# Reordered steps ahead of two chunks, GpSimd subtractions in pieces of 256 columns, and identity turns on TensorE

## Chip, cores and metric

The kernel runs on one core of a Trainium2 chip. The metric is the device time of one execution in microseconds (us), here the median of three runs.

## What is computed

Batch 4, 8 heads, 576 tokens, head width 64, model width 512. Local attention, a gated channel mix, a token mix of rank 32 and a two-layer network follow one another. Cut to what matters:

```python
# attention: plain window of 32 keys for heads 0-3, every 4th of 128 keys for heads 4-7
scores = where(masks, q @ k.T / sqrt(64), -1e9)
attn   = exp(scores - max); attn = attn / (sum(attn) + 1e-9)
x      = attn @ v                                   # [4, 576, 512]
# channel mix, widths 512 -> 1024 -> 512
x_prev = x shifted by one token (0 first)
xk = mu_k * x + (1 - mu_k) * x_prev
xr = mu_r * x + (1 - mu_r) * x_prev
x  = sigmoid(xr @ w_r) * (relu(xk @ w_k) ** 2 @ w_v)
# token mix of rank 32, then a network 512 -> 2048 -> 512
u   = x + (x.T @ U @ V).T
out = u + relu(u @ w_ch1) @ w_ch2
```

## The kernel before

Every matrix product of the two networks is made of three products of rounded parts: high by high, low by high, high by low (`three`, L1172 to L1174). So each operand has a high half (a rounded copy, made by ScalarE or GpSimd) and a low half (operand minus high half, made by VectorE or GpSimd).

**Attention** goes by parts and pairs. A part k is half a batch (256 or 320 tokens), a pair p two heads; "(1, 2)" is part 1, pair 2. Each has four steps:
- A: VectorE turns q and k in blocks of 32 (L951, L959).
- B: TensorE makes the scores (L1193, L1206); VectorE masks them and takes the maximum (L973, L979, L983); ScalarE takes the exponentials (`exps`, L720); VectorE normalises (`normalise`, L1006 to L1011).
- C: TensorE turns the probabilities against an identity matrix (L1213); ScalarE copies them out (L710).
- D: TensorE multiplies by v (L1224); VectorE copies the result into `x` (L993 to L997).

Part 0 and the scores of (1, 0) run ahead of everything, in the order of the list `BEFORE`; the others are dealt to slots by the tables `FIRST_ONE`, `SECOND_ONE` and `LATER`. Each engine's program writes its order out by hand.

**Channel mix** goes by nine chunks of 256 tokens. A chunk has ten units on TensorE, one slot of attention behind each: k units (128 columns of `xk @ w_k`) and two r units (128 tokens of `xr @ w_r`), in the order k0, k1, k2, r0, r1, k3 to k7. Behind some units stand the products with `w_v` (`V_AFTER`), which need the square of a k unit: ScalarE makes relu and the rounded square, VectorE the square (`sq`, L1030) and its low half (`sq_l`, L1034).

For the first chunk the k mix is made pair by pair: ScalarE shifts (`first_shift`), VectorE mixes (`mix`, L1020), ScalarE rounds (`high_first`), VectorE makes the low half (`low_first`, L1103). The r mix is made by GpSimd (`mix_r`, L633), rounded by ScalarE (`high_first_r`, L784), and its low half made by GpSimd (`low_first`, L644). In later chunks GpSimd makes the low half of the r mix in one instruction (`low_xr`, L628).

**Weights** come in pieces of 512 KB (`load_piece`); the first ten are split into halves by GpSimd (`split_both`, L621 and L622). Piece 0 serves k0 and k1, piece 1 k2 and k3, pieces 2 and 3 the r units, piece 4 the first products with `w_v`. The pieces of the last network are rounded by ScalarE and subtracted by GpSimd (`split_low`, L613).

**Queues.** SyncE issues q, v, most weights and a part of k, in program order, each load waiting for its buffer. ScalarE issues seven loads of k (`load_keys`). GpSimd goes through its splits, mixes and low halves in program order.

Of the kernel before, what the change touches and what calls it, by code (L numbers as in the profile page):

```python
# [30 lines left out]
D = H * DH  # L31
# [51 lines left out]
def blocks(k, p):  # L83
# [8 lines left out]
          ("D", 0, 2), ("C", 0, 3), ("D", 0, 3), ("B", 1, 0)]  # L92
NUNIT = 10

LATER = {"A": [-7, -5, -2, 0], "B": [-6, -4, -1, 1], "C": [-2, 0, 3, 5], "D": [-1, 1, 4, 6]}
FIRST_ONE = {"A": [None, None, 1, 2], "B": [None, 0, 1, 3], "C": [1, 3, 4, 5], "D": [2, 4, 5, 6]}
# [108 lines left out]
def build(nc, q, k_in, v, mu_k, mu_r, w_k, w_v, w_r, u_in, v_in, w_ch1, w_ch2, out):  # L205
    ctx = ExitStack()
    with ctx:
# [160 lines left out]
        def wait(eng, s, value):  # L368

            value = value + CREDIT.get(id(s), 0)  # L370
            if isinstance(value, int) and value <= 0:
                return
            eng.wait_ge(s, value)
# [13 lines left out]
        def two_of(step):  # L387
            return two_banks[TWO[GROUP[step]]]
# [67 lines left out]
        def _(sp):  # L456
# [71 lines left out]
            load_qk(0, 0)  # L528
            load_qk(0, 1)
            load_v(0, 0)  # L530
            load_qk(0, 2)
            load_piece(0)
            load_v(0, 1)
            load_qk(0, 3)
            load_piece(1)
# [3 lines left out]
            load_piece(2)  # L539
# [35 lines left out]
        def _(pool):  # L575
# [33 lines left out]
            def split_low(n):  # L609

                raw, hi, lo = piece(n)
                pool.wait_ge(w_hi, n - FIRST2 + 1)
                pool.tensor_tensor(lo, raw, hi.bitcast(F32), ALU.subtract).then_inc(w_split, 1)  # L613

            def split_both(n):

                raw, hi, lo = piece(n)
                pool.wait_ge(stage_in[slot_of(n)], STAGE_COUNT[n])
                half = raw.shape[1] // 2
                for a in (slice(0, half), slice(half, 2 * half)):  # L620
                    step(pool.tensor_copy(hi[:, a], raw[:, a]))  # L621
                    ins = pool.tensor_tensor(lo[:, a], raw[:, a], hi[:, a].bitcast(F32), ALU.subtract)  # L622
                ins.then_inc(w_split, 1)

            def low_xr(c):

                wait(pool, xrh_done, c + 2)
                pool.tensor_tensor(xs_l[:, 1], xf[:, 1], xs_h[:, 1].bitcast(F32), ALU.subtract).then_inc(xrl_done, 1)  # L628
# [12 lines left out]
            def low_first(half):  # L641
                wait(pool, xrh_done, half + 1)
                f = HEAD_PAIR[2 * half]
                return pool.tensor_tensor(xs_l[:, 1, f:f + 2], xf[:, 1, f:f + 2], xs_h[:, 1, f:f + 2].bitcast(F32), ALU.subtract)  # L644
# [18 lines left out]
            low_first(0)  # L663
            low_first(1).then_inc(xrl_done, 1)
            for n in range(4, NB_PIECES):
                split_both(n)
# [35 lines left out]
        def _(act):  # L702
# [110 lines left out]
            def chunk(c):  # L813
                last = c == NC1 - 1
                for n, (kind, m) in enumerate(UNITS):
# [12 lines left out]
                    if c == 0 and n == 2:  # L828
                        high_first_r(0)
                        high_first_r(1)  # L830
                    if n == NUNIT - 2 and c > 0 and not last:
                        high_x(1, c + 1)
                    if c < MIX_CHUNK:
                        attention_slot(c * NUNIT + n)
                    else:
                        for step in mix_steps("scalar", (c - MIX_CHUNK) * NUNIT + n):
                            mix_step(*step)
# [16 lines left out]
            def first_exps(k, p):  # L854
                exps(k, p, 0)
                exps(k, p, 1)
# [22 lines left out]
            load_keys(1, 0, range(2, 4))  # L879
            first_exps(0, 3)  # L880
            first_shift(1)
            attention("C", 0, 2)
            high_first(1)
            load_keys(1, 1)
            first_shift(2)
            attention("C", 0, 3)
# [4 lines left out]
            shift_for_r(0, 1)  # L891
            load_keys(1, 2)
            shift_for_r(0, 2)
# [34 lines left out]
        def _(dve):  # L928
# [140 lines left out]
            def chunk(c):  # L1069
                last = c == NC1 - 1  # L1070
                slot = c * NUNIT
                for n, (kind, m) in enumerate(UNITS):
                    if n >= 1 and UNITS[n - 1][0] == "k":
                        square(c, UNITS[n - 1][1])
                    for t in range(KT):
                        if not last and n == MIX_SLOT[c][t]:
                            mix(c + 1, t)
                    if c < MIX_CHUNK:
                        for step in steps_in(slot + n):
                            attention(*step)  # L1080
                        for k, p in normalised_in(slot + n):
                            normalise(k, p)
                    else:
                        for step in mix_steps("vector", (c - MIX_CHUNK) * NUNIT + n):
                            mix_step(*step)
# [37 lines left out]
            low_first(0)  # L1123
            mix(0, 1)
            normalise(0, 3)
            attention("D", 0, 2)
            low_first(1)
            mix(0, 2)
            attention("A", 1, 0)
# [5 lines left out]
            attention("A", 1, 1)  # L1135
            for c in range(NC1):
                chunk(c)
# [29 lines left out]
        def _(pe):  # L1167
# [7 lines left out]

            def attention(stage_, k, p):
# [5 lines left out]
                dst, run = two_of((stage_, k, p)), run_of((stage_, k, p))  # L1182
                every = units(k, p)
# [23 lines left out]
                elif stage_ == "C":  # L1207
                    if n == 0:
                        pe.wait_ge(consts, 1)
# [121 lines left out]

            pe.wait_ge(cleared, 2)
            for step in BEFORE:
                attention(*step)
            for n in range(len(BEFORE)):
                if TWO[n] < 2 and TWO[n] not in TWO[n + 1:]:
                    wait_drained(pe, GROUPS[n])
            for c in range(NC1):
                chunk(c)
# [65 lines left out]
```

## Time and profile before

| | |
|---|---|
| runs | 789.57, 789.8, 791.19 us; median 789.8 us |
| profiled execution | 787.75 us, of which the span from the first to the last instruction is 785.7 us |
| mean granted TensorE clock | 0.996 of full speed |
| busy | TensorE 95%, its weight loads 83%, VectorE 43%, ScalarE 38%, GpSimd 19% |
| DMA | 35.75 MB in 121746 packets |

Busy shares are means over stages with different limits: the first 50 us, with attention of part 0 and the first chunk, look different from the rest. In rows of the trace a time is counted from the start of the span. PE is TensorE, DVE VectorE, ACT ScalarE, POOL GpSimd, SP SyncE; SPq is SyncE's queue of DMA issues. In rows in order of time a bracket gives the idle time of the engine just ahead of the instruction, and what ended it.

### The profile page before, as it was taken

The page shows a single profiled execution, that of the slowest core. Times are in us where ns is not written, and L with a number is a line of the kernel's source. Part 1 is how long each engine was busy: PE and PEld are TensorE (multiplying, and loading weights), DVE is VectorE, ACT ScalarE, POOL GpSimd, SP SyncE. Part 2 cuts the span into 40 slices and gives each one's busy share as a digit, 9 for nine tenths or more (in the row PEclk, how much of TensorE's full clock was granted, in tenths as well). Part 3 has the DMA queues.
Part 4 walks back from the last instruction along what each step waited for, and adds up shares of the span by engine and source line. Part 5 has one row for each costly group of instructions (what it writes and reads, how often), then busy time and mean ns, then how long its engine had stood idle before and what let it go on. Part 6 is the DMA issues. An engine that isn't in the chain of part 4 may idle for free.

```text
span 785.7 us, 13228 instructions
## 1 busy us (share of the span) xinstructions
PE 749.7 (95%) x5020; PEld 655.0 (83%) x5020; DVE 334.5 (43%) x704; ACT 295.6 (38%) x777; POOL 149.9 (19%) x163
## 2 busy tenths in 40 slices
PE   4589899999999999989999999999999999999998
PEld 3467788888888887779889999899998989989997
DVE  6768776767676846755411311221131122113111
ACT  4657676666777665612532211111111111112110
POOL 5777220102011215200665000000000000000000
PEclk9989999999999999999999999999999999999999
DMA  7963342333233201000342100010010001001001
GB/s 143 208 155 61 65 82 48 60 57 70 42 59 62 56 1 54 1 27 1 113 143 67 41 0 1 1 40 0 0 40 0 0 0 40 0 0 41 0 1 41
DMA packets 121746, 35.75 MB, mean 46 GB/s; under 512 B 109536, under 2 KB 115680, under 8 KB 121696
## 3 DMA queue, kind: packets, MB, share of 16 engines
q1 hardware_dynamic: 112000, 34.02, 17.9%
q10 hardware_dynamic: 9696, 1.05, 0.9%
q8 instruction: 32, 0.52, 0.3%
q14 instruction: 18, 0.15, 0.1%
HBM read 30.33 MB, written 4.72 MB: 45 GB/s over the span
## 4 chain that ended last, share of the span: by engine, by line
PE 88%; DVE 7%; issue 2%; ACT 2%; ACTq 0%; POOL 0%; DMA 0%; DVEq 0%
PE bank L1172 27%; PE bank L1174 26%; PE bank L1173 26%; PE bank L1224 2%; PE bank L1193 2%; PE bank L1213 2%; DVE sq L1030 1%; PE bank L1253 1%; DVE xf L1020 1%; DVE probs L973 1%; PE bank L1314 1%; DVE sq_l L1034 1%; ACT probs L720 1%; DVE neg_max L983 1%; PE bank L1326 0%
## 5 line engine op out<-in xcount | busy, mean ns | idle before, releaser
L1142 DVE SCALAR_TENSOR_TENSOR h_l<-bank,h_h 128x384 fp32r<-128x384 f32 x96 | 53.5, 558 | 305.6 <-ACT h_h L912 305.5
L912 ACT ACTIVATE h_h<-bank 128x384 fp32r<-128x384 f32 x96 | 47.2, 492 | 330.7 <-PE bank L1174 330.7
L1172 PE MATMUL bank<-ut_h,w_h 128*128 128x384 f32 x384 | 130.6, 340 | 0.7 <-POOL w_l L613 0.7
L1174 PE MATMUL bank<-ut_h,w_l 128*128 128x384 f32 x384 | 129.3, 337 | 0.0
L1173 PE MATMUL bank<-ut_l,w_h 128*128 128x384 f32 x384 | 128.8, 336 | 0.0
L1174 PE MATMUL bank<-w_h,h_l 128*128 128x512 f32 x288 | 113.7, 395 | 0.0
L1173 PE MATMUL bank<-w_l,h_h 128*128 128x512 f32 x288 | 113.5, 394 | 0.0
L1172 PE MATMUL bank<-w_h,h_h 128*128 128x512 f32 x288 | 112.0, 389 | 0.0
L1172 PE MATMUL bank<-xs_h,wk_h 128*128 128x256 f32 x288 | 85.6, 297 | 1.9 <-DVE xs_l L1103 1.9
L1173 PE MATMUL bank<-xs_l,wk_h 128*128 128x256 f32 x288 | 81.1, 282 | 0.0
L1174 PE MATMUL bank<-xs_h,wk_l 128*128 128x256 f32 x288 | 80.9, 281 | 0.0
L1172 PEld LDWEIGHTS bank<-ut_h,w_h 128*128 128x128 f32 x384 | 72.2, 188 | 4.9 <-POOL w_l L613 1.0
L1173 PEld LDWEIGHTS bank<-ut_l,w_h 128*128 128x128 f32 x384 | 72.2, 188 | 3.0
L1174 PEld LDWEIGHTS bank<-ut_h,w_l 128*128 128x128 f32 x384 | 72.0, 188 | 0.0
L1172 PE MATMUL bank<-wv_h,sq_h 128*128 128x512 f32 x144 | 58.8, 408 | 5.1 <-DVE sq_l L1034 5.0
L1174 PEld LDWEIGHTS bank<-w_h,h_l 128*128 128x128 f32 x288 | 54.0, 188 | 11.5
L1173 PEld LDWEIGHTS bank<-w_l,h_h 128*128 128x128 f32 x288 | 54.0, 188 | 9.5
L1172 PEld LDWEIGHTS bank<-w_h,h_h 128*128 128x128 f32 x288 | 54.1, 188 | 9.0
L819 ACT ACTIVATE relu_k<-bank 128x256 f32<-128x256 f32 x72 | 27.0, 375 | 90.7 <-PE bank L1174 90.6
L1172 PEld LDWEIGHTS bank<-xs_h,wk_h 128*128 128x128 f32 x288 | 54.8, 190 | 5.8 <-issue 3.3
L1173 PE MATMUL bank<-wv_l,sq_h 128*128 128x512 f32 x144 | 57.0, 396 | 0.0
L1174 PE MATMUL bank<-wv_h,sq_l 128*128 128x512 f32 x144 | 56.9, 395 | 0.0
(118 smaller groups left out, 1211.9 us busy)
## 6 DMA issues: line engine op xcount, KB each, us to landing
stage<-in_moe_w_ch_dram SPq DMA_DIRECT2D x16, 512.0 KB, 3.4
out_dram<-result SPq DMA_DIRECT2D x18, 256.0 KB, 2.0
q_raw<-in_q_dram SPq DMA_DIRECT2D x64, 40.0 KB, 2.1
q_raw<-in_q_dram SPq DMA_DIRECT2D x64, 32.0 KB, 2.1
v_raw<-in_v_dram SPq DMA_DIRECT2D x32, 64.0 KB, 2.4
k_raw<-in_k_dram SPq DMA_DIRECT2D x48, 40.0 KB, 2.1
k_raw<-in_k_dram SPq DMA_DIRECT2D x52, 32.0 KB, 2.1
stage<-in_moe_w_k_dram SPq DMA_DIRECT2D x3, 512.0 KB, 4.1
```

Of the source, the lines that this page charges most:

```text
L720: ins = act.activation(probs[b][:, keys * i:keys * i + keys], probs[b][:, keys * i:keys * i + keys], ACT.Exp, bias=neg_max[:, b, i:i + 1], ...
L819: act.activation(relu_k[:, m % 2, :], unit_bank[n % 2][:, 0:C1], ACT.Relu).then_inc(unit_out, 1)
L912: act.activation(h_h[:, m % KRING, :], h_bank[m % 2][:, 0:C2], ACT.Relu).then_inc(hh_done, 1)
L973: ins = dve.scalar_tensor_tensor(probs[b][:, 0:4 * keys].rearrange("p (h c) -> p h c", h=2), banks[:, :, 0:2 * keys], DH ** -0.5, m[:, :, ...
L983: dve.tensor_reduce(neg_max[:, b, 0:nu], probs[b][:, 0:nu * keys].rearrange("p (a b) -> p a b", b=keys), op=ALU.max, axis=AX_X, negate=Tru ...
L1142: dve.scalar_tensor_tensor(h_l[:, m % KRING, :], h_bank[m % 2][:, 0:C2], 0.0, h_h[:, m % KRING, :].bitcast(F32), op0=ALU.max, op1=ALU.subt ...
L1172: pe.matmul(dst, lhs[0], rhs[0], start=start, stop=False)
L1173: pe.matmul(dst, lhs[0], rhs[1], start=False, stop=False)
L1174: return pe.matmul(dst, lhs[1], rhs[0], start=False, stop=stop)
L1193: ins = pe.matmul(dst[UQ * a:UQ * a + UQ, h, col:col + keys], q_t[n % 2][rows, query:query + UQ], k_t[p][rows, first_key:first_key + keys] ...
L1213: ins = pe.transpose(run[0:keys, i * P:i * P + P], probs[n % 2][:, keys * i:keys * i + keys], ident[:, :])
L1224: ins = pe.matmul(run[rows, to:to + wide], v_raw[n % VALUES][0:keys, i + a, rows], probs_t[n % 2][0:keys, block_, first:first + wide], sta ...
```

## The change

- `FIRST_ONE`: step A of (1, 2) goes ahead of chunk 0, and that of (1, 3) from slot 2 to slot 1.
- SyncE: pieces 0, 1 and 2 are loaded earlier than some loads of q and v.
- GpSimd: subtractions go in pieces of 256 columns (`split_low`, `split_both`, `low_xr`, `low_first`), and piece 4 is split ahead of the low half of the first r mix.
- ScalarE: other order of the steps ahead of chunk 0; in chunk 0 `high_first_r` goes from behind the relu of unit 2 to behind the attention slot of unit 1.
- VectorE: other order ahead of chunk 0; in chunk 0 (1, 0) is normalised ahead of the scores of (1, 1).
- TensorE: `keep_clock` turns the identity matrix into a bank that is free, 18, 12, 10, 6, 8, 3, 5 and 6 times ahead of seven attention steps and of chunk 0. It waits for the identity at the start.

```diff
+IDLE_TURNS = {("B", 0, 0): 18, ("B", 0, 1): 12, ("C", 0, 0): 10, ("B", 0, 3): 6, ("D", 0, 2): 8, ("C", 0, 3): 3, ("D", 0, 3): 5, "chunk": 6}
...
-FIRST_ONE = {"A": [None, None, 1, 2], "B": [None, 0, 1, 3], "C": [1, 3, 4, 5], "D": [2, 4, 5, 6]}
+FIRST_ONE = {"A": [None, None, None, 1], "B": [None, 0, 1, 3], "C": [1, 3, 4, 5], "D": [2, 4, 5, 6]}
...
             load_qk(0, 0)
+            load_piece(0)
             load_qk(0, 1)
             load_v(0, 0)
             load_qk(0, 2)
-            load_piece(0)
+            load_piece(1)
+            load_qk(0, 3)
             load_v(0, 1)
-            load_qk(0, 3)
-            load_piece(1)
+            load_piece(2)
             load_v(0, 2)
             load_v(0, 3)
             load_qk(1, 0)
-            load_piece(2)
             load_qk(1, 1)
             load_piece(3)
...
             def split_both(n):
...
-                half = raw.shape[1] // 2
-                for a in (slice(0, half), slice(half, 2 * half)):
+                raw, hi, lo = (a.rearrange("p t (z n) -> p (t z) n", n=256) for a in (raw, hi, lo))
+                for a in (slice(0, 2), slice(2, 4)):
                     step(pool.tensor_copy(hi[:, a], raw[:, a]))
-                    ins = pool.tensor_tensor(lo[:, a], raw[:, a], hi[:, a].bitcast(F32), ALU.subtract)
+                    for i in range(a.start, a.stop):
+                        ins = pool.tensor_tensor(lo[:, i], raw[:, i], hi[:, i].bitcast(F32), ALU.subtract)
...
             def low_xr(c):
 
                 wait(pool, xrh_done, c + 2)
-                pool.tensor_tensor(xs_l[:, 1], xf[:, 1], xs_h[:, 1].bitcast(F32), ALU.subtract).then_inc(xrl_done, 1)
+                for f in range(KT):
+                    ins = pool.tensor_tensor(xs_l[:, 1, f], xf[:, 1, f], xs_h[:, 1, f].bitcast(F32), ALU.subtract)
+                ins.then_inc(xrl_done, 1)
...
                 mix_r(0, t)
-            low_first(0)
-            low_first(1).then_inc(xrl_done, 1)
-            for n in range(4, NB_PIECES):
+            split_both(4)
+            for t in range(KT):
+                ins = low_first(t)
+            ins.then_inc(xrl_done, 1)
+            for n in range(5, NB_PIECES):
...
-                    if c == 0 and n == 2:
-                        high_first_r(0)
-                        high_first_r(1)
...
                         attention_slot(c * NUNIT + n)
+                        if c == 0 and n == 1:
+                            high_first_r(0)
+                            high_first_r(1)
...
             load_keys(1, 0, range(2, 4))
+            attention("C", 0, 2)
             first_exps(0, 3)
             first_shift(1)
-            attention("C", 0, 2)
+            load_keys(1, 1)
             high_first(1)
-            load_keys(1, 1)
+            attention("C", 0, 3)
             first_shift(2)
-            attention("C", 0, 3)
             high_first(2)
             shift_for_r(0, 0)
             first_shift(3)
             high_first(3)
             shift_for_r(0, 1)
+            shift_for_r(0, 2)
             load_keys(1, 2)
-            shift_for_r(0, 2)
...
                     if c < MIX_CHUNK:
+                        if slot + n == 0:
+                            normalise(1, 0)
                         for step in steps_in(slot + n):
                             attention(*step)
...
             low_first(0)
+            normalise(0, 3)
             mix(0, 1)
-            normalise(0, 3)
             attention("D", 0, 2)
             low_first(1)
+            attention("A", 1, 0)
             mix(0, 2)
-            attention("A", 1, 0)
...
             attention("A", 1, 1)
+            attention("A", 1, 2)
...
+            def keep_clock(ahead_of, scratch):
+                for _ in range(IDLE_TURNS.get(ahead_of, 0)):
+                    pe.transpose(scratch[:, 0:P], ident[:, :], ident[:, :])
...
                 dst, run = two_of((stage_, k, p)), run_of((stage_, k, p))
+                keep_clock((stage_, k, p), run)
...
+            pe.wait_ge(consts, 1)
             pe.wait_ge(cleared, 2)
...
+            keep_clock("chunk", unit_bank[0])
             for c in range(NC1):
                 chunk(c)
```

## Rows read from the trace of the kernel before

**Rows 1.** The page's busy times: us (share of the span) and instructions.

```profile
PE 749.7 (95%) x5020; PEld 655.0 (83%) x5020; DVE 334.5 (43%) x704; ACT 295.6 (38%) x777; POOL 149.9 (19%) x163
```

**Rows 2.** TensorE in order of time, 30 to 76 us: start, duration, instruction.

```profile
30.05 0.55 PE L1172 MATMUL bank<-xs_h,wk_h 128*128 128x256 f32 x1 [1.89 <-DVE xs_l L1103]
...
37.98 0.72 PE L1213 MATMUL bank<-ident,probs 128*96 128x128 f32 x5 [1.83 <-DVE probs L1011]
39.59 0.56 PE L1193 MATMUL bank<-k_t,q_t 64*64 64x96 f32 x16 [0.89 <-DVE k_t L951]
...
45.98 0.77 PE L1172 MATMUL bank<-wr_h,xs_h 128*128 128x512 f32 x1 [3.24 <-issue]
...
63.63 0.72 PE L1213 MATMUL bank<-ident,probs 128*96 128x128 f32 x5 [0.56 <-DVE probs L1011]
...
75.17 0.60 PE L1213 MATMUL bank<-ident,probs 128*64 128x128 f32 x4 [0.77 <-DVE probs L1011]
```

**Rows 3.** Windows: PE, PEld, DVE, ACT, POOL busy, then granted clock, DMA share, GB/s.

```profile
34.84:45.08 10.24, 5.18 (x72) 4.42 (x71) 8.91 (x24) 6.59 (x26) 4.18 (x6) 1.00 0.83 196
45.08:51.91 6.83, 5.93 (x14) 4.70 (x15) 3.45 (x3) 2.25 (x6) 6.59 (x7) 0.50 0.80 202
51.91:58.00 6.09, 6.09 (x46) 4.83 (x46) 3.44 (x8) 2.93 (x8) 5.85 (x7) 1.00 0.47 126
```

**Rows 4.** ScalarE in order of time: last exponential of (1, 1); the two roundings.

```profile
40.38 0.19 ACT L720 ACTIVATION_READ_ACCUMULATOR probs<-probs,neg_max 128x1 f32 x1
...
42.69 1.13 ACT L784 ACTIVATE xs_h<-xf 128x512 fp32r<-128x512 f32 x2
```

**Rows 5.** GpSimd in order of time: piece 3, r mix, its low half, piece 4.

```profile
30.88 0.61 POOL L621 CAST wr_h<-x 128x512 fp32r<-128x512 f32 x1
...
34.71 2.61 POOL L633 TENSOR_TENSOR xf<-xf,shifted 128x256 f32<-128x256 f32 x4
43.38 2.50 POOL L644 TENSOR_TENSOR xs_l<-xf,xs_h 128x512 fp32r<-128x512 f32 x2 [6.06 <-ACT xs_h L784]
45.82 1.04 POOL L621 CAST wv_h<-x 128x512 fp32r<-128x512 f32 x1
```

**Rows 6.** SyncE's queue in order of time: the issue of piece 3.

```profile
24.70 0.46 SPq L514 DMA_DIRECT2D x<-in_moe_w_r_dram  x1
```

**Rows 7.** DMA issues at 22 to 23 and 24.5 to 25 us: size, us to landing.

```profile
x<-in_moe_w_r_dram SPq DMA_DIRECT2D x1, 512.0 KB, 4.4
...
x<-in_moe_w_r_dram SPq DMA_DIRECT2D x1, 512.0 KB, 5.8
```

**Rows 8.** VectorE in order of time: q of (1, 0), q of (1, 2).

```profile
25.35 0.73 DVE L951 STREAM_TRANSPOSE q_t<-q_raw 128x256 f32<-128x256 f32 x2
...
38.55 0.50 DVE L951 STREAM_TRANSPOSE q_t<-q_raw 128x320 f32<-128x320 f32 x1
```

**Rows 9.** VectorE in order of time: squares and a low half.

```profile
80.12 2.59 DVE L1030 TENSOR_TENSOR sq<-relu_k 128x256 f32<-128x256 f32 x1
...
331.11 2.20 DVE L1030 TENSOR_TENSOR sq<-relu_k 128x256 f32<-128x256 f32 x1
333.35 2.52 DVE L1034 TENSOR_TENSOR sq_l<-sq,sq_h 128x256 fp32r<-128x256 f32 x1
...
336.38 0.41 DVE L1030 TENSOR_TENSOR sq<-relu_k 128x256 f32<-128x256 f32 x1
```

**Rows 10.** GpSimd in order of time, beside the rows before.

```profile
80.01 2.42 POOL L628 TENSOR_TENSOR xs_l<-xf,xs_h 128x1024 fp32r<-128x1024 f32 x1 [5.89 <-ACT xs_h L771]
...
330.63 2.41 POOL L628 TENSOR_TENSOR xs_l<-xf,xs_h 128x1024 fp32r<-128x1024 f32 x1 [1.17 <-ACT xs_h L771]
333.24 2.34 POOL L613 TENSOR_TENSOR w_l<-stage,w_h 128x1024 fp32r<-128x1024 f32 x1 [0.21 <-ACT w_h L738]
```

**Rows 11.** TensorE in order of time, at the same two places.

```profile
83.23 0.50 PE L1172 MATMUL bank<-wv_h,sq_h 128*128 128x512 f32 x1 [2.11 <-DVE sq_l L1034]
...
335.91 0.50 PE L1172 MATMUL bank<-wv_h,sq_h 128*128 128x512 f32 x1 [2.54 <-DVE sq_l L1034]
```

More of the change, by code:

```diff
@@ L612, in split_low @@
                 pool.wait_ge(w_hi, n - FIRST2 + 1)
-                pool.tensor_tensor(lo, raw, hi.bitcast(F32), ALU.subtract).then_inc(w_split, 1)
+                raw, hi, lo = (a.rearrange("p t (z n) -> p (t z) n", n=256) for a in (raw, hi, lo))
+                for i in range(4):
+                    ins = pool.tensor_tensor(lo[:, i], raw[:, i], hi[:, i].bitcast(F32), ALU.subtract)
+                ins.then_inc(w_split, 1)
             def split_both(n):
@@ L618, in split_both @@
                 pool.wait_ge(stage_in[slot_of(n)], STAGE_COUNT[n])
-                half = raw.shape[1] // 2
-                for a in (slice(0, half), slice(half, 2 * half)):
+                raw, hi, lo = (a.rearrange("p t (z n) -> p (t z) n", n=256) for a in (raw, hi, lo))
+                for a in (slice(0, 2), slice(2, 4)):
                     step(pool.tensor_copy(hi[:, a], raw[:, a]))
-                    ins = pool.tensor_tensor(lo[:, a], raw[:, a], hi[:, a].bitcast(F32), ALU.subtract)
+                    for i in range(a.start, a.stop):
+                        ins = pool.tensor_tensor(lo[:, i], raw[:, i], hi[:, i].bitcast(F32), ALU.subtract)
                 ins.then_inc(w_split, 1)
@@ L639, in make_xr, with low_first @@
                 low_xr(c)
[L641 to L644, printed above, removed]
+            def low_first(t):
+                wait(pool, xrh_done, t // 2 + 1)
+                f = HEAD_PAIR[t]
+                return pool.tensor_tensor(xs_l[:, 1, f], xf[:, 1, f], xs_h[:, 1, f].bitcast(F32), ALU.subtract)
             pool.memset(u_pad[:, :, :, :].rearrange("p a t r -> p (a t r)"), 0.0).then_inc(u_zero, 1)
@@ L1081, in chunk @@
                         for k, p in normalised_in(slot + n):
-                            normalise(k, p)
+                            if (k, p) != (1, 0):
+                                normalise(k, p)
                     else:
@@ L1207, in attention @@
                 elif stage_ == "C":
-                    if n == 0:
-                        pe.wait_ge(consts, 1)
                     wait(pe, normed, n + 1)
```

## The prediction

> **What bounds the kernel now.** I read the page's busy times first, then TensorE in order of time, then GpSimd, SyncE and ScalarE over the first 50 us, and at the end VectorE against GpSimd. TensorE is busy for 749.7 us of a 785.7 us span [rows 1]: 36.0 us are all that can be gained by removing its waits, and what a faster clock gives comes on top. The profiled execution took 787.75 us, 2.05 us less than the median of the three runs (789.8 us) and below the lowest of them. I work out differences on the profiled execution and take them off the median.
>
> The reader should look at TensorE's order of time [rows 2]. Chunk 0 begins at 30.05 us. Inside it TensorE waits 1.83 us for the normalised probabilities of part 1, pair 0, then 0.89 us for the turned q and k of pair 2, then 3.24 us ahead of the first r unit at 45.98 us. Behind that it waits 0.56 and 0.77 us at two turns of probabilities, and later twice for the low part of a square [rows 11]. The granted clock belongs to the same stretch [rows 3]: it is at 2.4 GHz (1.00) from 34.84 us, falls to 1.2 GHz (0.50) at 45.08 us, which is inside the gap of 3.24 us, and comes back at 51.91 us, after 5.93 us of work at half speed. That work lost 5.93 / 2 = 2.96 us.
>
> So the start of the first r unit is the place to price. What sets it? It needs the low half of the r mix. GpSimd made that at 43.38 us, after 6.06 us of waiting for ScalarE's rounding (high_first_r), which ran at 42.69 us because it stood behind the relu of unit 2 [rows 4, 5].
>
> **The first r unit after the change: 3.4 us earlier.** Two chains must both end.
>
> GpSimd's chain: its piece 3 is issued by SyncE at 24.70 us [rows 6]. Before piece 3 the queue holds the same loads in both kernels, piece 2 included, only in another order, so I leave the issue at 24.7. It landed 5.8 us after the issue; piece 2 landed 4.4 us after its own [rows 7]. With piece 2's 512 KB out of the way earlier, I take 4.8 us, landing at 29.5 us (bounds 29.1 and 30.5). Piece 3's split lasts from 30.88 to 34.71 us, 3.83 us [rows 5]; GpSimd waits for the data now, since the earlier pieces come early, so it ends at 33.4. Four mixing sums take 2.6 us [rows 5]: 36.0. The new order puts the split of piece 4 here, another 3.9 us with two more instructions: 39.9. Four low parts of 256 columns cost what four mixing sums of that size cost, 2.6 us: 42.5. The unit starts 0.1 us later, at 42.6.
>
> ScalarE's chain: the two roundings come behind the exponentials of pair 1, which end at 40.57 us in the trace of before [rows 4]. Chunk 0 starts about a microsecond earlier (below), so I expect them at about 39.5 to 40.6; at the old time they would end at 40.57 + 1.13 = 41.7 us [rows 4] and the unit would start at about 43.1. GpSimd's chain therefore decides, with 42.2 to 43.6 as bounds from the landing, and 44.0 if a rounding is late as well. The gain is 45.98 - 42.6 = 3.4 us, bounds 2.0 and 3.8.
>
> **Edits that I cost at nothing, and their cover.** Normalising pair 0 of part 1 ahead of pair 1's scores, and turning pair 2 ahead of the chunk, take away the 1.83 and 0.89 us waits. Even without them and with the old start TensorE would only reach the first r unit at (45.98 - 3.24) - 2.72 = 40.0 us, where it waits until 42.6: they are covered by GpSimd's chain, and would be worth 2.7 us if that chain ended first. The moved turn is one more thing that VectorE waits for: pair 2's k is loaded by ScalarE's queue after one more shift. The normalising, the scores and the squares of the chunk stand behind it. It was done at 38.55 us [rows 8], so a late landing has cover only while these stay ahead of ScalarE's roundings.
>
> In the preamble, piece 0 now goes ahead of q of pair 1, piece 1 ahead of q of pair 3 and piece 2 ahead of two loads of v. Each may hold the small loads for one transfer. The turn of part 1's first q and k goes ahead of mix 2 on VectorE; in the kernel before it ran at 25.35 us right behind that mix [rows 8], so its data had landed by then, and at worst VectorE waits for it until about 25.35. The mix, the turn and the low parts after it then end 0 to 1 us before the old time. So chunk 0 starts between 29.0 and 30.05 us. TensorE's slack of 2.6 us at the r unit covers all of this.
>
> The 68 identity turns: one turn costs 0.72 - 0.60 = 0.12 us at full clock (five turns against four [rows 2]) and twice that at half, together 8.2 to 16.3 us. They stand where TensorE waits, ahead of steps whose operands are late. Where a turn outlasts its wait (12 turns at half clock are 2.9 us) the preamble moves by some tenths, which VectorE's wait for q and k covers. The Trainium skill (TensorE: Matmul & The Clock Gate, Part 4: PE-mode transpose) says that transpose mode does not engage the full clock as other matmuls do. No row of the kernel before has turns alone ahead of a rise, so the trace shows neither. By that rule the sum is unchanged, since no term rests on the turns; without it the second case below would be likelier by about a tenth.
>
> **The clock at the r unit: nothing gained.** If TensorE reaches the r unit at 39 to 40 and starts at 42.6, it stands still for 2.6 to 3.6 us. The nearest row is the 3.24 us gap, in which the clock fell. I take the same half-speed stretch again: 0, with 2.96 us as the upper bound and a loss of 0.5 as the lower (a stretch that begins a little later relative to the unit).
>
> **GpSimd's subtractions in pieces of 256 columns: 4.1 us.** Beside GpSimd's 1024-column subtraction at 80.01 us (2.42 us), VectorE's square took 2.59 us [rows 9, 10], where the same shape takes 0.41 [rows 9]: 2.2 us of it were GpSimd's. TensorE then waited 2.11 us for the low part of that square [rows 11]. In four pieces a VectorE instruction is held for one piece, 2.42 / 4 = 0.6 us. Held on the square and again on its low part, VectorE still gains 2.2 - 1.2 = 1.0 us; held on neither, all 2.11. I take 1.3.
> At 331 us it happens twice in a row: the square takes 2.20 us beside one subtraction, its low part 2.52 beside the next [rows 9, 10], 3.9 us in excess. With at most 0.6 for each, 2.7 us go, more than TensorE's wait of 2.54 [rows 11]. I take 2.4 (1.5 to 2.54).
> The waits of 0.56 and 0.77 us [rows 2] end chains on VectorE in the stretch where GpSimd splits weights without a pause; with halved holds I take 0.4 of them (0 to 1.3). The added instructions cost GpSimd a few hundredths each, and it idles from there on.
>
> **Sum.** 3.4 + 0 + 1.3 + 2.4 + 0.4 = 7.5 us: 789.8 - 7.5 = 782.3 us. TensorE is busy almost throughout after the first r unit, so a shift there should survive to the end.
>
> **The rivals.** About 0.2% (1.6 us) is what a measurement of this kernel can tell from no change.
> - Half speed again at the r unit, as forecast: 782.3 us, its own range 780 to 785, chance 0.52.
> - The clock stays at 2.4 GHz through the gap, since the units before it are packed more closely: 2.96 us more, 779.3 us. For it: an idle stretch of 1.83 us in the kernel before did not lower the clock [rows 2, 3]. Against it: 3.24 did. Chance 0.26.
> - A new wait takes the place of the old one: pair 2's turn stands ahead of the chunk and its k lands late, VectorE's queue stands still, ScalarE's roundings slip to the old time, and the r unit starts near 45.5 us. Only the finer pieces remain: 789.8 - 4.1 - 0.5 = about 785.2 us. Chance 0.11.
> - No measurable change: VectorE is held by every piece in turn and nothing is gained at the squares, and what the r unit gains is given back to VectorE later in chunk 0. About 789 us, chance 0.06.
> - Slower: with the r unit earlier, waits between the next units keep the clock at 1.2 GHz through chunk 0. Each microsecond at half speed loses half a microsecond, so this eats the 7.5 us when the low stretch reaches 6.83 + 15 = 21.8 us, and is slower by 0.2% from 25 us on. A stretch of 31 us gives 789.8 - 7.5 + 12.1 = 794.4 us. Against it: in the kernel before the clock came back 5.93 us into the r unit although the stretch began idle [rows 3]. Chance 0.05.
>
> **How the numbers follow.** Faster by over 0.2%: 0.52 + 0.26 + 0.11 = 0.89; within 0.2%: 0.06; slower: 0.05. The range reaches down to the second case with larger gains at the squares (777.5 us) and up past the third (786 us); the last two cases, and the extreme ends of the others, are left out.
>
> **What would show it.** TensorE's first r unit should start at 42 to 44 us, released by GpSimd's low part; the piece ahead of it should be the split of piece 4. The waits of 1.83 and 0.89 us should be gone. The granted clock shows 0.50 somewhere between 42 and 52 us in the first case and not in the second. Squares near 77 and 326 us should take under 1.1 us. The prediction is wrong if the r unit starts after 45 us, if the waits for the low part of a square stay above 1.5 us, or if TensorE shows new waits of more than 2 us in chunk 0 or 1.

## The result and the profile after

The kernel after the change takes 783.78 us (median of five runs, 782.64 to 784.97), the kernel before beside it 790.93 us (789.57 to 792.81). The ratio is 0.991 [0.9889, 0.993], that is 7.1 us less. The profiled execution of after took 783.19 us, its span 781.4 us.

Busy times of after, to be read against [rows 1]:

```profile
PE 756.1 (97%) x5088; PEld 661.5 (85%) x5088; DVE 328.6 (42%) x704; ACT 295.2 (38%) x777; POOL 168.4 (22%) x257
```

TensorE has 68 instructions more, the turns. GpSimd has 94 more and is busy for 18.5 us longer. TensorE of after in order of time, against [rows 2, 11]:

```profile
31.04 0.39 PE L1187 MATMUL bank<-xs_h,wk_h 128*128 128x256 f32 x1 [1.59 <-DVE xs_l L1117]
...
38.90 0.72 PE L1231 MATMUL bank<-ident,probs 128*96 128x128 f32 x5 [2.54 <-DVE probs L1022]
...
46.94 0.77 PE L1187 MATMUL bank<-wr_h,xs_h 128*128 128x512 f32 x1 [2.49 <-issue]
...
63.10 0.72 PE L1231 MATMUL bank<-ident,probs 128*96 128x128 f32 x5 [0.39 <-DVE probs L1022]
...
73.84 0.60 PE L1231 MATMUL bank<-ident,probs 128*64 128x128 f32 x4 [0.17 <-DVE probs L1022]
...
80.69 0.50 PE L1187 MATMUL bank<-wv_h,sq_h 128*128 128x512 f32 x1 [0.89 <-DVE sq_l L1045]
```

The first r unit, which the forecast put at 42.6 us, starts at 46.94 us, a microsecond later than in the profile of before. The wait of 1.83 us for the probabilities of (1, 0) has not gone; it is now 2.54 us. Behind the r unit the waits shrink about as forecast: 0.56, 0.77 and 2.11 us have become 0.39, 0.17 and 0.89, and the 2.54 us near 335 us have no successor.

VectorE of after, in order of time, shows why the probabilities are late, and what the squares take, against [rows 8, 9]:

```profile
36.57 0.51 DVE L962 STREAM_TRANSPOSE q_t<-q_raw 128x320 f32<-128x320 f32 x1 [2.82 <-DMA k_raw<-in_k_dram]
37.01 0.47 DVE L962 STREAM_TRANSPOSE k_t<-k_raw 128x320 f32<-128x320 f32 x1
37.40 0.13 DVE L1017 TENSOR_SCALAR sums<-sums 128x5 f32<-128x5 f32 x1
...
78.80 0.97 DVE L1041 TENSOR_TENSOR sq<-relu_k 128x256 f32<-128x256 f32 x1
...
330.97 0.41 DVE L1041 TENSOR_TENSOR sq<-relu_k 128x256 f32<-128x256 f32 x1
331.42 0.85 DVE L1045 TENSOR_TENSOR sq_l<-sq,sq_h 128x256 fp32r<-128x256 f32 x1
```

The turn of (1, 2), which now stands ahead of the chunk, waits 2.82 us for k. The normalising of (1, 0) stands behind it and begins at 37.40 us. The three lower rows answer to squares of 2.59 and 2.20 us and a low half of 2.52 us before.

From there the delay goes through ScalarE to GpSimd. ScalarE's two roundings in after, then GpSimd, against [rows 4, 5]:

```profile
42.89 1.14 ACT L795 ACTIVATE xs_h<-xf 128x512 fp32r<-128x512 f32 x2
```

```profile
29.78 0.76 POOL L627 CAST wr_h<-x 128x512 fp32r<-128x512 f32 x1 [4.54 <-DMA x<-in_moe_w_r_dram]
...
34.28 2.61 POOL L642 TENSOR_TENSOR xf<-xf,shifted 128x256 f32<-128x256 f32 x4
...
39.97 1.59 POOL L629 TENSOR_TENSOR wv_l<-x,wv_h 128x256 fp32r<-128x256 f32 x2
43.58 3.26 POOL L653 TENSOR_TENSOR xs_l<-xf,xs_h 128x256 fp32r<-128x256 f32 x4 [2.02 <-ACT xs_h L795]
...
78.69 4.20 POOL L636 TENSOR_TENSOR xs_l<-xf,xs_h 128x256 fp32r<-128x256 f32 x4 [5.69 <-ACT xs_h L782]
```

GpSimd has done the split of piece 4 at 41.56 us and waits 2.02 us for the roundings. The last row is the subtraction that took 2.42 us in one instruction [rows 10]: in four pieces it takes 4.20 us. The shortest of the 32 pieces of this kind in after takes 0.72 us, so four of them would be 2.9 us; the other 1.3 us fall where VectorE works beside them, whose square and low half take 0.97 and 0.83 us there instead of 0.41 and 0.42.

How can the time fall by 7 us when the r unit starts later than in the profile of before? That profile isn't the typical execution. A second one has its first r unit at 48.31 us (below). Over the 59 executions of before that ran beside the experiments time goes roughly with the mean granted clock: 0.996 in seven of them, 788.3 us on average; 0.993 in 19, 789.9 us; 0.989 in seven, 791.8 us. The profile of before, with 0.996, is one of the short ones.

The table gives, for one profiled execution of each kernel, the start of the first and the second r unit of chunk 0, of the first r unit of chunk 1, and the rest of the span from there. Kernels are compared below by their ratios to runs of before on the same chip, with the 95% interval in brackets.

| kernel | r0 | r1 | r0 of chunk 1 | rest | span |
|---|---|---|---|---|---|
| before | 45.98 | 54.23 | 90.61 | 695.1 | 785.7 |
| before, again | 48.31 | 56.30 | 92.49 | 695.0 | 787.5 |
| after | 46.94 | 53.87 | 88.43 | 693.0 | 781.4 |
| e1 pieces only | 48.91 | 55.95 | 92.34 | 693.0 | 785.3 |
| e2 whole subtractions | 44.30 | 52.09 | 87.88 | 695.1 | 783.0 |
| e3 no turns | 46.20 | 54.22 | 88.74 | 692.9 | 781.6 |
| e7 turns only | 47.11 | 55.16 | 91.72 | 695.1 | 786.8 |
| e4 turn in slot 1 | 44.92 | 52.34 | 86.69 | 692.9 | 779.6 |
| e5 old loads | 47.34 | 55.47 | 90.09 | 692.9 | 783.0 |
| e6 both | 46.64 | 53.65 | 88.27 | 692.9 | 781.2 |
| e8 slot 1, more turns | 44.75 | 51.85 | 86.39 | 692.9 | 779.3 |
| e9 early keys | 44.82 | 52.53 | 86.52 | 693.0 | 779.5 |
| e10 keys and turns | 44.56 | 50.15 | 85.35 | 693.1 | 778.4 |
| e11 three edits | 43.17 | 50.68 | 86.78 | 693.0 | 779.8 |

Two things can be read off. The rest takes one of two values: 695.0 to 695.1 with whole subtractions (four profiles), 692.9 to 693.1 with pieces (ten), whatever else is changed. And against the second profile of before the 6.1 us of span are 1.4 up to the first r unit, 1.1 more up to the second, 1.6 up to chunk 1's, and 2.0 behind it.

### The profile page after: what moved, and what is told of

Same layout as the page of the kernel before. It is cut to its first block, busy times and chain, and to the rows that moved or that the text cites. A ratio compares the mean times of both kernels' runs of the same rounds, so it can differ in the third digit from the quotient of the medians.

```text
span 781.4 us, 13455 instructions
## 1 busy us (share of the span) xinstructions
PE 756.1 (97%) x5088; PEld 661.5 (85%) x5088; DVE 328.6 (42%) x704; ACT 295.2 (38%) x777; POOL 168.4 (22%) x257
## 4 chain that ended last, share of the span: by engine, by line
PE 88%; DVE 5%; issue 2%; ACT 2%; DMA 1%; SPq 0%; POOL 0%; ACTq 0%; DVEq 0%
PE bank L1187 27%; PE bank L1189 26%; PE bank L1188 26%; PE bank L1242 2%; PE bank L1231 2%; PE bank L1213 2%; PE bank L1271 1%; PE bank L1332 1%; DVE sq L1041 1%; DVE probs L984 1%; PE bank L1344 1%; DMA q_raw<-in_q_dram 1%; DMA k_raw<-in_k_dram 1%; ACT probs L731 1%; DVE sq_l L1045 0%
## 5 line engine op out<-in xcount | busy, mean ns | idle before, releaser
L618 POOL TENSOR_TENSOR w_l<-stage,w_h 128x256 fp32r<-128x256 f32 x64 | 47.7, 777 | 46.2 <-ACT w_h L749 46.1
```

The costliest lines, as they stand in the source:

```text
L618: ins = pool.tensor_tensor(lo[:, i], raw[:, i], hi[:, i].bitcast(F32), ALU.subtract)
```

## The experiments

The letters in the expectations stand for what is said to carry the gain or the wait: P the pieces, O the orders, T the turns on TensorE, C the clock at the r unit, W VectorE's wait for k of (1, 2), L the moved loads as the cause of a late start, G GpSimd's chain, S the three edits of e11 alone.

**Pieces alone (e1) and all but the pieces (e2).** e1 is the kernel before with the finer subtractions in `split_low`, `split_both`, `low_xr` and `low_first`; e2 is the kernel after with these four as before. The edit of e1, at one of the four places:

```diff
-                pool.tensor_tensor(lo, raw, hi.bitcast(F32), ALU.subtract).then_inc(w_split, 1)
+                raw, hi, lo = (a.rearrange("p t (z n) -> p (t z) n", n=256) for a in (raw, hi, lo))
+                for i in range(4):
+                    ins = pool.tensor_tensor(lo[:, i], raw[:, i], hi[:, i].bitcast(F32), ALU.subtract)
+                ins.then_inc(w_split, 1)
```

> The kernel before with one part of the change alone: GpSimd's subtractions in pieces of 256 columns. Theory P (the pieces carry the gain): TensorE's waits of 2.11 and 2.54 us at the squares shrink to under 1 us and 0, those of 0.56 and 0.77 us by about half, and the time falls by 4 to 5 us; the first r unit stays at about 46 us. Rival O (orders and turns carry it): less than 1.5 us faster, since VectorE is only held by the next piece instead.

> The changed kernel with GpSimd's subtractions whole again, all orders and turns as changed. Theory P: only 2 to 3 us faster than the kernel before, with both waits at the squares back at over 2 us. Rival O: 6 to 7 us faster, as the whole change.

Measured: e1 0.9961 [0.9945, 0.9977], 3.1 us faster; e2 0.9965 [0.9951, 0.9979], 2.8 us faster. So both halves of the change are real and of about one size. TensorE of e1, at new and old waits:

```profile
79.79 0.56 PE L1200 MATMUL bank<-k_t,q_t 64*64 64x96 f32 x16 [1.21 <-DVE k_t L958]
...
84.93 0.50 PE L1179 MATMUL bank<-wv_h,sq_h 128*128 128x512 f32 x1 [1.12 <-DVE sq_l L1041]
```

and of e2:

```profile
80.48 0.50 PE L1180 MATMUL bank<-wv_h,sq_h 128*128 128x512 f32 x1 [2.12 <-DVE sq_l L1038]
...
333.32 0.50 PE L1180 MATMUL bank<-wv_h,sq_h 128*128 128x512 f32 x1 [2.53 <-DVE sq_l L1038]
```

With whole subtractions both old waits are back to within a hundredth of a microsecond. With pieces the second has gone and the first is halved, but in e1 a wait of 1.21 us for a turn on VectorE takes the place of what the first gave: from the second r unit to chunk 1's, e1 takes 36.4 us and before 36.2 to 36.4.

**No turns (e3), and the turns alone in the kernel before (e7).**

```diff
-IDLE_TURNS = {("B", 0, 0): 18, ("B", 0, 1): 12, ("C", 0, 0): 10, ("B", 0, 3): 6, ("D", 0, 2): 8, ("C", 0, 3): 3, ("D", 0, 3): 5, "chunk": 6}
+IDLE_TURNS = {}
```

> The changed kernel without the 68 identity turns. Theory T (the turns raise the clock, which fell again twice near the first r unit): TensorE's steps before 30 us run at half speed, chunk 0 starts about 1 us later than with turns, and the kernel is 0.5 to 2 us slower than the changed one. Rival (the start of chunk 0 hangs on loads and VectorE alone, so the turns are worth nothing): within 0.5 us of the changed kernel.

> The kernel before with the 68 identity turns alone. Theory T: the granted clock is 1.00 from about 6 us on, chunk 0 starts 1 to 2 us earlier, the units k0 and k1 take 1.4 us each instead of 2.6 and 1.8, but the first r unit still waits for its low half, and the time falls by 1 to 2.5 us. Rival (worth nothing): within 0.8 us of the kernel before.

Measured: e3 783.2 us, 0.992 [0.9902, 0.9938], no different from after; e7 1.0005 [0.999, 1.002]. The turns are worth nothing that these runs can tell. They do act on TensorE, though. After, then e3, at the first steps:

```profile
1.54 4.10 PE L1193 MATMUL bank<-ident 128*128 128x128 f32 x18 [1.54 <-POOL ident L589]
6.73 0.46 PE L1213 MATMUL bank<-k_t,q_t 64*64 64x64 f32 x16 [1.09 <-DVE k_t L970]
7.12 1.53 PE L1193 MATMUL bank<-ident 128*128 128x128 f32 x12
```

```profile
5.76 0.71 PE L1213 MATMUL bank<-k_t,q_t 64*64 64x64 f32 x16 [5.76 <-DVE k_t L970]
```

18 turns with nothing beside them take 4.10 / 18 = 0.23 us each. The 16 scores behind them take 0.46 us, against 0.71 without turns, and the next twelve turns 0.13 us each. (That these scores start a microsecond later in after than in e3 is not the turns' doing: VectorE waits 4.26 us for the first k in after and 3.20 in e3, with the same loads.) But the scores begin when VectorE has turned k, and so does all that follows: a quarter of a microsecond gained in a chain that hangs on loads goes into the next wait. Chunk 0 starts at 29.97 us in e7, and at 30.05 and 30.16 in the two profiles of before.

**The wait for k (e4) and the moved loads (e5, e6), beside another profile of before.** e4 leaves the turn of (1, 2) in slot 1, as in the kernel before; e5 gives SyncE's loads their old order; e6 does both.

```diff
-FIRST_ONE = {"A": [None, None, None, 1], "B": [None, 0, 1, 3], "C": [1, 3, 4, 5], "D": [2, 4, 5, 6]}
+FIRST_ONE = {"A": [None, None, 1, 1], "B": [None, 0, 1, 3], "C": [1, 3, 4, 5], "D": [2, 4, 5, 6]}
...
             attention("A", 1, 1)
-            attention("A", 1, 2)
```

> The changed kernel with one edit taken back: q and k of part 1, pair 2 are turned in slot 1 of chunk 0 again and not ahead of the chunk (those of pair 3 stay in slot 1). Theory W (the new wait of VectorE for k of pair 2, 2.8 us in the trace of the changed kernel, is what ate the earlier start of the first r unit): the normalising of pair 0 starts about 2 us earlier, ScalarE's roundings end near 41 instead of 44 us, the first r unit starts at 44 to 45 us instead of 46.9, and the kernel is 1.5 to 2.5 us faster than the changed one. Rival G (GpSimd's own queue holds the r unit anyway): within 0.5 us of the changed kernel.

> The changed kernel with SyncE's loads in the order of before. Theory L (piece 0 ahead of the small loads made the first q and k land 1.1 to 2 us later): the first turn starts at 4.5 us instead of 5.6, the second at 7.4 instead of 9.3, chunk 0 starts near 29 us instead of 31.0, the first r unit at 44 to 45 us, and the kernel is 1.5 to 3 us faster than the changed one. Rival G: the pieces then come later, GpSimd's splits end later, and the time is within 0.5 us of the changed kernel or worse.

> The changed kernel with both edits taken back: loads in the order of before, and the turn of pair 2 in slot 1. Theories W and L together: the first r unit at 43.5 to 44.5 us, where GpSimd's queue holds it, and 2 to 3.5 us faster than the changed kernel. Rival G: no more than 0.5 us.

> The kernel before once more, for a second profile: the first was 2 to 3 us below the median of its runs. If the clock's place relative to the first r unit varies, this one shows a low stretch at another time and the first r unit up to 3 us later; if not, the same rows with a difference outside the span.

Measured: e4 781.24 us (780.5 to 781.83), 0.9885 [0.9866, 0.9905]; e5 783.92 us, 0.9918 [0.99, 0.9936]; e6 782.89 us, 0.9908 [0.989, 0.9926]; before 789.6 us in its one run, which fits its clock of 0.993. By the ratios e4 is 2.0 us faster than after; the two intervals overlap, but every run of e4 is below every run of after (before took 790.66 us beside e4 and 790.93 beside after), and the spans differ by 1.8 us. ScalarE, then GpSimd in e4:

```profile
40.85 1.14 ACT L795 ACTIVATE xs_h<-xf 128x512 fp32r<-128x512 f32 x2
```

```profile
41.54 2.98 POOL L653 TENSOR_TENSOR xs_l<-xf,xs_h 128x256 fp32r<-128x256 f32 x4 [0.56 <-ACT xs_h L795]
```

The roundings come 2.04 us earlier than in after and the r unit 2.02 us earlier, at 44.92. So the wait for k did hold the r unit. In e4 GpSimd is done at 44.52 us; the last 0.4 us are TensorE's own, which multiplies by v until then (1.50 us, against 0.89 in after). GpSimd and VectorE in e5, with the old loads:

```profile
36.62 2.97 POOL L642 TENSOR_TENSOR xf<-xf,shifted 128x256 f32<-128x256 f32 x4
...
43.88 3.36 POOL L653 TENSOR_TENSOR xs_l<-xf,xs_h 128x256 fp32r<-128x256 f32 x4
```

```profile
33.60 0.51 DVE L962 STREAM_TRANSPOSE q_t<-q_raw 128x320 f32<-128x320 f32 x1 [0.67 <-DMA k_raw<-in_k_dram]
```

Chunk 0 of e5 starts at 30.21 us instead of 31.04, and TensorE reaches the r unit early; but GpSimd, fed later, goes from mix to split to low half without a pause, and the r unit starts at 47.34 us after 7.06 us of idle time. Between these two profiles the moved loads cost the preamble 0.8 us and let GpSimd end its mix 2.7 us earlier (36.89 against 39.59). Over all profiles chunk 0 starts at 30.03 to 31.39 us with the moved loads and at 29.58 to 30.59 with the old ones, seven of each. L has fallen, G holds, and e6 says the same: both edits are taken back in it, yet GpSimd goes without a pause again, its low half ends at 46.54 us, and the r unit starts at 46.64 and not at 43.5 to 44.5. e4 and e6 differ by the loads alone and ran on one chip: with the wait for k gone the moved loads are worth 1.65 us (781.24 against 782.89, every run of e4 below every run of e6).

The wait for k is short in e5, 0.67 us, and it is not of one length with the moved loads either: 2.82 us in after, 1.91 in e3, 0.28 in the profile of e2, where the r unit then starts at 44.30. In after and e3 the last of the four loads of this k is issued just behind SyncE's load of piece 4 (32.10 behind 32.05 us, 31.65 behind 31.51), and VectorE goes on 4.5 and 4.2 us later; in e2 and e5 it is issued ahead of piece 4 (31.32 ahead of 32.22, 31.04 ahead of 33.86), and VectorE goes on 2.5 and 2.6 us later. Four profiles fit the reading that the big load delays the small one; it wasn't tried by itself.

The second profile of before shows what the first hides. TensorE in it:

```profile
37.52 0.72 PE L1213 MATMUL bank<-ident,probs 128*96 128x128 f32 x5 [1.98 <-DVE probs L1011]
...
39.98 0.92 PE L1193 MATMUL bank<-k_t,q_t 64*64 64x96 f32 x16 [1.74 <-DVE k_t L951]
...
48.31 0.76 PE L1172 MATMUL bank<-wr_h,xs_h 128*128 128x512 f32 x1 [3.65 <-issue]
```

and its windows, columns as in [rows 3]:

```profile
40.30:43.00 2.70, 2.70 (x28) 2.48 (x21) 1.62 (x5) 0.00 (x0) 0.00 (x0) 0.50 0.74 169
43.70:46.50 2.80, 0.97 (x26) 0.78 (x24) 2.61 (x8) 2.59 (x9) 1.19 (x1) 1.00 0.63 166
47.00:53.00 6.00, 4.69 (x11) 3.75 (x12) 2.21 (x3) 1.83 (x5) 5.76 (x7) 0.50 0.74 176
```

The clock falls twice, at the two waits ahead of it and at the r unit. In its first profile [rows 3] the first of these falls is missing: the scores ahead of unit 2 took 0.56 us there and 0.92 here, and the r unit starts 2.3 us later here. ScalarE shows the way from one to the other:

```profile
43.88 0.38 ACT L819 ACTIVATE relu_k<-bank 128x256 f32<-128x256 f32 x1 [3.77 <-PE bank L1174]
44.30 0.42 ACT L789 ACTIVATE sq_h<-relu_k 128x256 fp32r<-128x256 f32 x1
44.62 1.13 ACT L784 ACTIVATE xs_h<-xf 128x512 fp32r<-128x512 f32 x2
```

The roundings stand behind the relu of unit 2, which waits for TensorE's slow unit, and come 1.93 us later than in the first profile [rows 4]. In after they stand ahead of it, so a low clock in unit 2 no longer reaches the r unit by this path.

**The keys earlier (e9).** e9 keeps the turn ahead of the chunk and loads its k earlier on ScalarE's queue.

```diff
             load_keys(1, 1)
+            load_keys(1, 2)
             high_first(1)
...
             shift_for_r(0, 2)
-            load_keys(1, 2)
             shift_for_r(0, 3)
```

> The changed kernel with k of part 1, pair 2 loaded right behind that of pair 1 on ScalarE's queue, the turn still ahead of the chunk. Theory W (it was the landing of this k that cost 2.8 us): VectorE's wait there is gone, the normalising of pair 0 starts about 2 us earlier, the first r unit at 44 to 45 us, and the kernel is 1.5 to 2.5 us faster than the changed one. Rival: TensorE then stands still longer ahead of the r unit and its clock falls for longer, so that less than 0.8 us is gained.

Measured: 781.36 us (780.92 to 781.58), 0.9887 [0.9868, 0.9907], as e4; it is 1.8 us faster than after by the ratios, with overlapping intervals and every run below every run of after. VectorE turns (1, 2) at 33.51 us without a wait, and GpSimd doesn't pause any more once piece 3 has landed:

```profile
30.00 0.61 POOL L627 CAST wr_h<-x 128x512 fp32r<-128x512 f32 x1 [4.96 <-DMA x<-in_moe_w_r_dram]
...
34.19 3.04 POOL L642 TENSOR_TENSOR xf<-xf,shifted 128x256 f32<-128x256 f32 x4
...
41.57 3.15 POOL L653 TENSOR_TENSOR xs_l<-xf,xs_h 128x256 fp32r<-128x256 f32 x4
```

This is the chain of the forecast, step by step: piece 3 at 30.0 us instead of 29.5, its split and the mix done at 37.2 instead of 36.0, piece 4 at 41.6 instead of 39.9, the low half at 44.7 instead of 42.5, the unit at 44.82 instead of 42.6.

**More turns, to hold the clock (e8, e10).** e8 is e4 with 20 turns ahead of the scores of (1, 2). e10 is e9 with 24 turns ahead of the first r unit (an entry of 24 in `IDLE_TURNS`, and this):

```diff
+                        if c == 0 and m == 0:
+                            keep_clock("r", v_bank[0])
                         if m == 0:
                             wait(pe, xrl_done, c + 1)
```

> As the run with the turn of pair 2 in slot 1, with 20 more identity turns ahead of the scores of (1, 2), where TensorE waited 3.1 us there before its clock fell. Theory C (the clock at the first r unit is worth up to 3 us, as the half-speed stretch of 6.8 us says): the granted clock stays at 1.00 through 42 to 49 us, the first r unit still starts at about 44.9 us, the second follows 5 us later instead of 7.4, and the kernel is 1.5 to 2.5 us faster than with the turn in slot 1 alone. Rival N (turns do not hold the clock, or what the r units gain is lost to waits behind them): within 0.5 us of it.

> The run with the early load of k, with 24 identity turns ahead of the first r unit into a bank that is free there. Theory C: the clock stays at 1.00 through the first r unit, the second r unit follows 5 us behind the first, 2 to 3 us faster than with the early load alone. Rival N: within 0.5 us of it.

Measured: e8 780.91 us, 0.9884 [0.9863, 0.9904]; e10 780.48 us (780.25 to 782.05), 0.9881 [0.9861, 0.9901], the lowest median of all. In e8 the clock fell at the r unit all the same (0.58 on average from 45.4 to 48.9 us). In e10 it did not; e9, then e10, same window, columns as in [rows 3]:

```profile
42.39:49.21 6.82, 4.39 (x10) 3.47 (x11) 4.33 (x8) 2.72 (x10) 6.66 (x10) 0.53 0.77 197
```

```profile
42.39:49.21 6.82, 5.64 (x32) 4.51 (x30) 4.81 (x8) 3.66 (x12) 6.66 (x9) 1.00 0.73 196
```

From the first r unit to the second e10 takes 5.59 us and e9 7.71, so 2.1 us are gained there. TensorE of e10 behind it:

```profile
59.41 0.72 PE L1231 MATMUL bank<-ident,probs 128*96 128x128 f32 x5 [0.42 <-DVE probs L1022]
...
70.75 0.60 PE L1231 MATMUL bank<-ident,probs 128*64 128x128 f32 x4 [0.78 <-DVE probs L1022]
```

e9 has neither wait. At the second r unit e10 is 2.4 us ahead; at chunk 1's r unit 1.2 us of it are left, and 0.9 in the medians, which the intervals do not separate from nothing. Of the 2 to 3 us that were expected no more is shown.

**Three edits alone (e11).** The kernel before with the pieces, the normalising of (1, 0) first in slot 0, and the roundings of the r mix behind slot 1; loads, turns, the split of piece 4 and the preamble stay as before.

```diff
+                        if slot + n == 0:
+                            normalise(1, 0)
                         for step in steps_in(slot + n):
                             attention(*step)
...
-                    if c == 0 and n == 2:
-                        high_first_r(0)
-                        high_first_r(1)
...
                         attention_slot(c * NUNIT + n)
+                        if c == 0 and n == 1:
+                            high_first_r(0)
+                            high_first_r(1)
```

> The kernel before with three parts of the change alone: GpSimd's pieces of 256 columns, pair 0 of part 1 normalised ahead of the scores of pair 1, and the two roundings for the r mix behind slot 1. No turns, no other loads, no other order ahead of chunk 0, piece 4 split where it was. Theory S (these three carry the change): the roundings end near 41 us, the first r unit starts at 43.5 to 45 us, and the kernel is 6 to 9 us faster than before, no slower than the changed one. Rival (the moved turns and loads are needed): 3 to 5 us faster, little more than the pieces alone.

Measured: 782.28 us (781.61 to 782.96), 0.9914 [0.9894, 0.9934]: these three edits give as much as the whole change. TensorE of e11:

```profile
39.23 0.56 PE L1203 MATMUL bank<-k_t,q_t 64*64 64x96 f32 x16 [2.80 <-DVE k_t L958]
...
43.17 0.47 PE L1182 MATMUL bank<-wr_h,xs_h 128*128 128x512 f32 x1 [0.79 <-issue]
...
47.90 0.49 PE L1182 MATMUL bank<-wv_h,sq_h 128*128 128x512 f32 x1 [1.71 <-POOL wv_l L626]
...
79.38 0.50 PE L1182 MATMUL bank<-wv_h,sq_h 128*128 128x512 f32 x1 [1.12 <-DVE sq_l L1041]
```

Its r unit starts earliest of all kernels, since GpSimd does not split piece 4 ahead of the low half; the 1.71 us at 47.90 are the price, as that split is late now. The wait of 2.80 us for the turn of (1, 2) stands where the moved turn, fed in time as in e9, has none.

## Why the prediction was right, and which step of it failed

**The time and the sign were right:** 782.3 us were forecast (777.5 to 786.0), 783.78 came; 7.5 us of gain, and 7.1.

**The r unit was wrong,** the largest term. "GpSimd's chain therefore decides", with the unit at 42.6 us, failed: ScalarE's roundings decided, at 42.89 us instead of 39.5 to 40.6, because the moved turn waited for k. The text priced this as its third case, "pair 2's turn stands ahead of the chunk and its k lands late", at 0.11, with the r unit near 45.5 us and a time of about 785.2. That mechanism took place; e4 and e9, which remove it in two ways, gain 2.0 and 1.8 us by the ratios. Its price did not hold: the case gave 4.6 us of gain (789.8 - 785.2) and 7.1 came, so more than the finer pieces remained. The sentence that "a late landing has cover only while these stay ahead of ScalarE's roundings" was the right test, and its answer was not looked for: k of (1, 2) is issued on ScalarE's queue behind a third shift, and the trace of before had no row that put its landing ahead of the chunk. What it had put the landing near 33.0 us: the last of its four loads was issued at about 30.3 us, with about 2.7 us to landing, and VectorE was done with the turn of (1, 1) at 32.62, so that a wait of some tenths could be read there. In after the last one is issued at 32.10 us and VectorE goes on at 36.57.

**Two errors in opposite directions.** That the sum came out is luck: the unit starts 4.3 us later in after than forecast, but in another profile of before it starts at 48.31 us, not 45.98. The 2.05 us between profile and median were taken as an offset that both kernels share. They go with the clock: over the executions of before 788.3 us at 0.996 and 789.9 at 0.993. The five executions of after show no such relation (783.78 us at 0.985, 784.08 at 0.993), but five are few.

**GpSimd's chain was right in order and 2.2 us too short.** In e9, where it decides, each step is longer than forecast (3.04 against 2.6 us for the mix, 3.15 against 2.6 for the low half, 4.2 and 4.4 for the splits of pieces 3 and 4 against 3.9), and the landing is 0.5 us later: piece 3 is issued at 25.50 us there and not at 24.7, and lands 4.5 us after that. Part of it is the price of cutting: "Four low parts of 256 columns cost what four mixing sums of that size cost" gave 2.6 us, and four of the shortest pieces take 2.9. That VectorE's work beside GpSimd makes up the rest fits; it wasn't tried by itself. So even without the wait for k the term is 3.5 us only against the second profile of before (48.31 - 44.82), and 1.2 against the first.

**The pieces:** 4.1 us forecast, 3.1 measured (1.8 to 4.3 by the interval). The 2.4 us at 331 us were 2.1 by the rest of the span: TensorE's 2.54 us of waiting there went, and its wait for GpSimd's low half `w_l` at 373 us grew from 0.70 to 1.12 us, 2.54 - 0.42 = 2.1; the 1.3 at 80 us were 2.11 - 0.89 = 1.2 in after, and nothing in e1, where VectorE is late elsewhere; the 0.4 at the two turns of probabilities were (0.56 + 0.77) - (0.39 + 0.17) = 0.8 in after, and 0.1 in e1. "A few hundredths each" for the added instructions was wrong: GpSimd is busy for 18.5 us longer with 94 more, 0.2 us each. Behind chunk 0 it has the time, but for the 0.42 us at `w_l`.

**The edits costed at nothing.** The turns: right, by e3 and e7. The Trainium skill (TensorE: Matmul & The Clock Gate, Part 4: PE-mode transpose) says that the full clock doesn't engage for transpose mode. The trace doesn't agree for the turns as this kernel issues them: 0.23 us each in the first 18, 0.13 in the next twelve. Normalising first and the earlier turn were not free: the first is in the set of e11 that gives as much as the whole change, the second cost about 2 us until its k came in time. The moved loads were no zero but effects that cancel in after (e5 takes as long): 0.8 us lost ahead of the chunk and a longer wait for k, against 2.7 us won on GpSimd's chain, which after can't use while it waits for ScalarE. Once it can, in e4 against e6, they are worth 1.65 us.

**The clock:** "the same half-speed stretch again" was right in that the clock of after still falls to 0.50 at the r unit, and wrong in the length: it is back at 1.00 about 3 us into the unit instead of 5.93, and from the first r unit to the second after takes 6.93 us, the two profiles of before 8.25 and 7.99. So 1.1 to 1.3 us come between the two r units in this one profile; in e3 the same stretch takes 8.02 us. It falls once more ahead of that, behind the wait of 2.54 us; this costs the r unit nothing, which waits for the roundings. Windows of after:

```profile
40.00:43.00 3.00, 3.00 (x29) 2.78 (x30) 2.93 (x6) 2.50 (x12) 1.57 (x2) 0.50 0.86 225
43.40:46.30 2.90, 1.05 (x26) 0.80 (x25) 2.79 (x8) 2.87 (x13) 2.72 (x4) 1.00 0.75 200
46.80:49.70 2.90, 2.76 (x7) 2.21 (x8) 2.75 (x5) 1.03 (x1) 2.82 (x5) 0.50 0.87 240
50.20:58.00 7.80, 7.80 (x54) 6.16 (x54) 3.50 (x8) 3.72 (x8) 7.56 (x11) 1.00 0.46 117
```

The bound of 2.96 us was not reached: with the clock held by turns (e10) the r unit gave 2.1 us at the place and 0.9 in the medians, which is not shown to differ from nothing.

**Open:** which of e11's two orders gives more, since they were not run apart; why the last load of k takes 2.5 us in some profiles and 4.5 in others; whether e4, e8, e9 and e10 differ among themselves; and whether e11's r unit at 43.17 us can be had together with a split of piece 4 that isn't late.

## What to carry to other kernels

An instruction that is moved ahead of others takes its wait with it: before costing it at nothing, find the issue and the landing of its operand, and what stands behind it in the queue; here 2.82 us of VectorE ahead of a normalising cost about 2 us of the end. A long instruction of GpSimd beside short ones of VectorE that TensorE waits for was worth cutting here, even though the cut made GpSimd slower. And the profile of before should be placed among its runs by granted clock and time before differences are read off it: the first r unit of one of the shortest executions started 2.3 us earlier than that of another.

## What the runs showed of the hardware

- Identity turns with nothing beside them raise TensorE's speed: in after 0.23 us each in the first 18, 0.13 in the next twelve, and scores of 0.46 us instead of 0.71. When it rises differs: of the nine profiles with these turns the first scores take 0.46 us in seven and 0.70 and 0.71 in two (e8, e10); the second scores take 0.46 in all nine, and 0.70 or 0.71 in e3 and in both profiles of before, which have no turns. Eight turns of after at 21.04 us took 1.83 us, also 0.23 each, and the granted clock was 0.50 (1.2 GHz) on average from 16.0 to 22.4 us; so the first 18 ran as at that level, though the clock's column reads 1.00 over them.
- A subtraction on GpSimd and an instruction of VectorE beside it hold each other up, and shorter ones for less long: four subtractions of 256 columns took 4.20 us beside VectorE's square, where one of 1024 took 2.42, and the square fell from 2.59 to 0.97 us. Cutting has its own price: the shortest piece takes 0.72 us, four 2.9, the shortest whole subtraction 2.34 [rows 10].
- Where the clock falls differs between executions of one kernel: once at the r unit in the first profile of before, twice in the second, with 2.3 us between their r units.
